# Filler transposes at the start, weights rounded earlier, and VectorE's row maximum moved ahead of the sum of P*V, in a fused attention and two-MLP kernel

## The reference, cut to what matters

```python
scores = scale * q @ k.T                      # 576 x 576 for each of 32 heads
thresh = max(scores, -1) - tau
scores = where(scores >= thresh, scores, -1e9)
attn   = exp(scores - max); attn /= (sum(attn) + 1e-9)
x      = attn @ v                             # then heads side by side: 2304 x 512
h = x @ w_in;  x = (h * sigmoid(1.702 * h)) @ w_out          # first MLP
h = x @ w_in2; out = (h * tanh(softplus(h))) @ w_out2        # second MLP
```

## Time and profile before

| | |
|---|---|
| median of 3 runs | 1164.55 us (1164.22 to 1164.59) |
| the profiled execution's own time | 1164.05 us |
| its span | 1162.3 us |
| granted TensorE clock, mean | 0.995 |
| busy: TensorE matmul / VectorE / ScalarE / GpSimd | 1118.1 / 759.1 / 724.1 / 295.4 us |

### The profile page before, as it was taken

One profiled execution on the slowest core, in us unless ns is written; L12 is line 12 of the kernel. 1 busy time (PEld: TensorE's weight loads), 2 busy tenths in 40 slices (PEclk: granted clock), 3 DMA queues, 4 the chain that ended last, 5 costly groups with the idle time before them and its releaser, 6 DMA issues.

```text
span 1162.3 us, 19359 instructions
## 1 busy us (share of the span) xinstructions
PE 1118.1 (96%) x7472; PEld 1035.4 (89%) x7472; DVE 759.1 (65%) x1359; ACT 724.1 (62%) x995; POOL 295.4 (25%) x502
## 2 busy tenths in 40 slices
PE   8978889999999999999999999999999999999998
PEld 4568889998999999999999999998999989899997
DVE  4678788888888888888888434665433444344343
ACT  3678787767777777777767322467545554554453
POOL 3557674434444433344333000000000000000000
PEclk9989999999999999999999999999999999999999
DMA  2443534232143222233231003520010000000000
GB/s 65 140 131 114 158 86 111 59 94 85 48 111 91 64 82 77 79 105 83 70 103 28 26 19 106 190 76 28 6 49 1 28 28 28 28 28 28 1 28 27
DMA packets 92923, 78.71 MB, mean 68 GB/s; under 512 B 47520, under 2 KB 78752, under 8 KB 92832
## 3 DMA queue, kind: packets, MB, share of 16 engines
q1 hardware_dynamic: 92832, 77.49, 22.9%
HBM read 63.83 MB, written 13.63 MB: 67 GB/s over the span
## 4 chain that ended last, share of the span: by engine, by line
PE 78%; DVE 11%; ACT 7%; issue 3%; POOL 0%; DMA 0%; SPq 0%; ACTq 0%; DVEq 0%
PE ps_s L743 17%; PE ps_r L628 14%; PE ps_r L648 11%; PE ps_r L766 9%; PE ps_t L492 6%; PE ps_t L513 5%; PE ps_t L766 4%; PE ps_s L477 4%; PE ps_t L648 3%; PE ps_r L513 2%; PE ps_s L466 2%; DVE x_pair L585 2%; DVE pt_lo L574 2%; ACT pv_half_sb L544 1%; DVE neg_max L554 1%
## 5 line engine op out<-in xcount | busy, mean ns | idle before, releaser
L628 PE MATMUL ps_r<-x_hi,wi_lo 128*128 128x256 f32 x544 | 158.5, 291 | 2.7 <-DVE x_lo L701 2.7
L810 DVE COPY hidden<-ps_s 128x768 f32<-128x768 f32 x48 | 45.8, 956 | 170.5 <-PE ps_s L743 170.5
L628 PE MATMUL ps_r<-x_lo,wi_hi 128*128 128x256 f32 x544 | 154.2, 284 | 0.0
L628 PE MATMUL ps_r<-x_hi,wi_hi 128*128 128x256 f32 x544 | 154.2, 283 | 0.0
L492 PE MATMUL ps_t<-ident,e_buf 128*128 128x128 f32 x720 | 118.1, 283 | 27.1 <-DVE pt_lo L574 14.5
L839 ACT ACTIVATE m_lo_raw<-m_lo_raw 128x1536 f32<-128x1536 f32 x24 | 35.8, 1491 | 168.8 <-DVE m_lo_raw L817 168.8
L561 DVE SCALAR_TENSOR_TENSOR e_buf<-ps_s,neg_thr,e_buf 128x576 f32<-128x576 f32 x144 | 117.0, 813 | 29.4 <-ACT e_buf L521 22.9
L648 PE MATMUL ps_r<-g_hi,wo_lo 128*128 128x256 f32 x464 | 135.4, 292 | 0.0
L537 ACT CAST pt_hi<-ps_t 128x640 fp32r<-128x640 f32 x128 | 89.0, 695 | 71.8 <-PE ps_t L492 69.6
L743 PE MATMUL ps_s<-x_hi,wi_lo 128*128 128x384 f32 x384 | 129.0, 336 | 2.4 <-DVE x_lo L799 2.4
L492 PEld LDWEIGHTS ps_t<-ident,e_buf 128*128 128x128 f32 x720 | 84.7, 143 | 52.1 <-issue 29.2
(11 more groups left out here) (105 smaller groups left out, 3009.9 us busy)
## 6 DMA issues: line engine op xcount, KB each, us to landing
k_ll_raw<-in_k SPq DMA_DIRECT2D x56, 288.0 KB, 2.9
v_st_raw<-in_v SPq DMA_DIRECT2D x64, 160.0 KB, 2.9
wi_lo_raw<-in_moe_w_in SPq DMA_DIRECT2D x16, 512.0 KB, 3.8
wo_lo_raw<-in_moe_w_out SPq DMA_DIRECT2D x16, 512.0 KB, 4.8
q_raw<-in_q SPq DMA_DIRECT2D x32, 192.0 KB, 2.9
x_scratch<-y_acc SPq DMA_DIRECT2D x9, 512.0 KB, 3.2
x_lo_raw<-x_scratch SPq DMA_DIRECT2D x6, 768.0 KB, 4.7
out_rows<-rows_out SPq DMA_DIRECT2D x18, 256.0 KB, 2.1
```

Of the source, the lines that this page charges most:

```text
L628: mm = pe.matmul(bank[:, part * CH:(part + 1) * CH], wi[w][:, k, f * P:(f + 1) * P], x[:, k, :], start=t == 0, stop=t == 3 * KT - 1)
```

## The change

Six edits:

1. TensorE starts with 12 transposes of the identity onto itself into an unused corner of a PSUM bank, and issues 3 more at the end of each of the turns 0 to 3 (`pe_idle`).
2. The weights' turns move from 9, 12, 14, 17, 19, 21, 23, 24, 26, 28, 30, 31, 33, 34, 36, 37 to 4, 6, 8, 10, 12, 14, 16, 18, 21, 23, 26, 28, 30, 31, 34, 35. The load is issued three turns ahead instead of four. VectorE subtracts the first seven, not four.
3. Chunk 0's first half stands in turn 18, not 19. The plan of turns 20 to 36 shifts by at most one half. From turn 37 it is the same.
4. In turn 18 ScalarE does the P*V copy and the rounding of x before `act_p_hi`.
5. VectorE subtracts the last of the four x blocks in turn 18, not 19.
6. In every turn with a group from 19 on, VectorE takes the maximum of step n before the sum of P*V.

```diff
-READY = [GROUPS[g][4] + (4 if c == 0 else 8) for c, g in enumerate(CHUNK_GROUP)]
+READY = [GROUPS[g][4] + (3 if c == 0 else 8) for c, g in enumerate(CHUNK_GROUP)]
...
-        W_SLOT = dict(zip((9, 12, 14, 17, 19, 21, 23, 24, 26, 28, 30, 31, 33, 34, 36, 37), W_ORDER))
+        W_SLOT = dict(zip((4, 6, 8, 10, 12, 14, 16, 18, 21, 23, 26, 28, 30, 31, 34, 35), W_ORDER))
...
-        W_FIRST = 4
+        W_FIRST = 7
...
+        def pe_idle(pe, count):
+
+            for _ in range(count):
+                pe.transpose(ps_r[:, 1, 384:512], ident[:, :], ident[:, :])
...
             pe.wait_ge(s["ident_ready"], 1)
+            pe_idle(pe, 12)
             pe_scores(pe, 0)
...
+                    if n < 4:
+                        pe_idle(pe, 3)
                     continue
...
-                    if n >= 2:
+                    if 2 <= n < FRONT + 2:
                         act_p_hi(act, n - 2)
...
                         act_x_hi_first(act, X_HI_FIRST[n])
+                    if n == FRONT + 2:
+                        act_p_hi(act, n - 2)
...
+                if 0 <= n < N:
+                    dve_max(dve, n)
                 if n >= FRONT + 3 and n - 3 in GROUP_AT:
                     dve_pv(dve, GROUP_AT[n - 3])
-                if 0 <= n < N:
-                    dve_max(dve, n)
...
-                if n - 1 in X_HI_FIRST:
-                    dve_x_lo_first(dve, X_HI_FIRST[n - 1])
+                for late in (1, 0):
+                    if n - late in X_HI_FIRST and (X_HI_FIRST[n - late] < KT - 1) == (late == 1):
+                        dve_x_lo_first(dve, X_HI_FIRST[n - late])
...
-                if n + 4 in W_SLOT:
-                    w_load(sp, 0, W_SLOT[n + 4])
+                if n + 3 in W_SLOT:
+                    w_load(sp, 0, W_SLOT[n + 3])
```

## The result

The changed kernel is slower: 1171.17 us in the median of 4 runs (1170.8 to 1173.82) against 1164.55 us. The ratio is 1.0064 with a 95% interval of 1.0053 to 1.0076, and the difference is 6.6 us. The profiled execution has a span of 1169.6 us, 7.3 us more than before. I had forecast 1165.6 us, between 1155 and 1173.

What follows compares the result with a forecast made beforehand. From 164 to 640 us TensorE's work plus its waits bound the kernel; the first 164 us hold most idle time. 1164.05 - 4.9 + 4.6 - 2.2 - 5.9 + 9.5 = 1165.15 us, 1165.6 as median; range 1155 to 1173.

Steps and rivals of the forecast that it cites:

- one of its own signs: The prediction is wrong if the first 86 us are not shorter by about 5 us.
- The other sign: From 164 to 640 us TensorE's idle time grows by 7 to 8 us; wrong if that stretch gets no longer.
- Edit 1: Filler transposes at the start lift TensorE's clock, so turn 5 starts at 20.8 us, not 25.66; gain 4.9 us.
- my rival: Transposes do not lift the clock at the start: 4.9 us gain becomes 2.5 us loss, 1173.0 us; chance 0.18.
- mask 0 would end near 9.3 us, mask 3 three loops later: First turns: with the clock up, VectorE's 2.67 us loop sets the pace, and mask 3 ends at 17.3 us.
- Edit 2, the front: Turns 4 to 18: weight roundings behind even turns' P*V delay the next exponential; loss 4.6 us.
- The term for turn 16: Turn 16's weight rounding stands ahead of the norm and copy that turn 18's P*V waits for; loss 1.04 us.
- The middle: Turns 21 to 37: three fewer weights at 0.74 us each; gain 2.2 us.
- Edits 3 to 5: Chunk 0: the 2.67 us wait and the half pace behind it go; gain 5.9 us.
- Edit 6: Maximum before sum delays 32 of 54 sums by 12.6 us, with 3.1 us won back; net loss 9.5 us.

Runs made afterwards that it cites:

- e12: e10 without turn 4's fillers, plus the maximum ahead of the sum only in 27 groups where VectorE had idle time; 1154.1 us, ratio 0.9915 to the kernel before.
- e5: The kernel before with 60 identity transposes ahead of the first scores; one run, 1168.18 us.
- e2: The changed kernel with edit 6 undone, the sum of P*V ahead of the maximum again; 1166.84 us, ratio 1.0032 to the kernel before.
- e3: The changed kernel with edit 2 undone, weights in their old turns and loads four turns ahead; 1166.65 us, ratio 1.0023 to the kernel before.
- e9: e8 with the change's fillers back (12, then 3 in each of turns 0 to 3); 1159.66 us, ratio 0.9963 to the kernel before.
- e10: e8 with fillers: 12 at the start, 12 ending turn 0, 6 ending each of turns 1 to 4; 1154.58 us, ratio 0.992 to the kernel before.
- e6: The kernel before with 40 fp32 matmuls on 64 of 128 rows ahead of the first scores; one run, 1178.21 us.
- e8: e7 with the first eight weights moved to odd turns 5 to 19, no fillers, sum first; 1158.67 us, ratio 0.9954 to the kernel before.
- e7: The kernel before with edits 3 to 5 alone; 1161.66 us, ratio 0.998 to the kernel before.
- e4: The kernel before with edit 6 alone, the maximum ahead of the sum; 1168.96 us, ratio 1.004 to the kernel before.
- e1: The changed kernel without edit 1's filler transposes; 1171.21 us, ratio 1.0058 to the kernel before.

## Why the prediction was right and wrong

The range held the time, in its upper part. The point, 1165.6 us, was no change that a measurement can tell, and 5.6 us too low; I had given slower a chance of 0.36 and faster 0.40. By one of its own signs the prediction failed: the first 86 us were to be about 5 us shorter, and the first sum, which stood at 86.14 us, came 3.4 us later. The other sign held in direction: TensorE's idle time from 164 to 640 us grew, by 4.4 us instead of 7 to 8. The terms one by one:

**Edit 1 is the step that failed.** I had put a gain of 4.9 us; the changed trace has a loss of 1.75 us at turn 5, near the 2.5 us of my rival. In that trace the twelve fillers did not lift the clock (4.18 us for the eight scores), as the rival had it, nor did they in e12's. But the rival's reason, that transposes cannot do it, is wrong. They can: 60 of them in e5, and 12 in the profiled executions of e2, e3, e9 and e10. The changed kernel, e2 and e3 start with the same instructions of TensorE, so the same start goes either way. Work on 64 rows does not lift it: e6 kept it low for 17.4 us, and so the scores are what left it low in the earlier trace rows, most likely. e5 and e6 differ in the operation as well as in the rows, but the P*V, a product on 128 rows, lifts it in every trace where it was low. What I never asked is what holds it. At full pace the scores end sooner, mask 0 does not, and TensorE idles 1.9 us where it had idled 0.73; in e2 and e3 the clock fell in that wait and stayed low until behind the first P*V, 28 us. My step "mask 0 would end near 9.3 us, mask 3 three loops later" took the clock as up, from the first scores on and for good. e10 puts nine more transposes into that gap (and three more into each of the next turns, six into turn 4), and there turn 5 starts at 21.19 us, where the sum had 20.8; e9's one good run had 20.43. That the added fillers are worth 4 us over e8 and 5 over e9 in the median is shown. Whether they do it by ending the idle time, by adding work on 128 rows, or by a second chance to lift the clock (e12) stays open: no run separates these. The Trainium skill's sentence on the PE-mode transpose ("TensorE: Matmul & The Clock Gate"), that it does not count as busy in the same way, is not what e5 shows: the pace of the transposes themselves doubled.

**Edit 2, the front**, had the mechanism right and the size partly by luck: 4.6 us forecast, 4.8 more lag between turn 5 and turn 18. The weights account for 3.6 us of it, the waits named behind turns 4, 6, 8 and 10 (0.84, 0.95, 0.85 and 0.95 more than before). e3 confirms the place and e8 the reason: the same roundings in odd turns cost next to nothing. The term for turn 16, "a full 1.04", was wrong: e3 and e5 have no weight in turn 16, and their P*V of turn 18 waits as long as that of the changed kernel. The rest is chance. In the changed trace the P*V of turn 12 ran at half pace and cost 1.7 us. In the old one that of turn 16 did, and it hid waits behind it:

```profile
62.14 4.06 PE L513 MATMUL ps_r<-pt_hi_raw,v_st_raw 128*64 128x256 f32 x10
...
68.62 2.37 PE L513 MATMUL ps_r<-pt_raw,v_st_raw 128*64 128x256 f32 x10 [0.67 <-ACT pt_raw L537]
```

In e5, whose turns are those of the kernel before behind the 60 fillers, the P*V of turn 16 is fast and the next one waits longer:

```profile
72.30 2.37 PE L513 MATMUL ps_r<-pt_raw,v_st_raw 128*64 128x256 f32 x10 [1.16 <-ACT pt_raw L537]
```

From turn 5 to turn 18 e5 takes 44.70 us and the kernel before 45.27, so the slow P*V of turn 16 cost only 0.6 us, and the two slow ones do not cancel. **The middle** was forecast at 2.2 us. e2 against the kernel before shows 1.6, with edits 3 to 5 in it; e3 against the changed kernel, which differ in the weights alone, shows 0.2.

**Edits 3 to 5** went the way described: no wait of 2.67 us, no fall of the clock there. The size was 5.9 us and turned out 3.1 (lag 6.57 at turn 18, 3.43 at the first sum), 3.2 in e7's trace; e7 gives 2.5 in the median. What I left out is of two kinds. Before the first sum 36 matmuls of the first MLP now stand where 24 stood, which takes one half, 1.4 us, more; and in e7 TensorE waits 0.95 us for the remainder of P in turn 20, where it had not waited. That half is one fewer later on, but e7's lead does not grow behind the first sum. It falls to 1.04 us at 141 us, of which 1.5 us are the fall of the clock at 110 us; why the missing half brings nothing there is not shown.

**Edit 6** had the right sign and mechanism and twice the size: 9.5 forecast, 4.3 in the median by e2 and 4.6 by e4. The mis-sized term is the time that the maximum adds ahead of the sum, 0.66 us and not the 0.77 from start to start; over the 54 sums that makes 9.2 us instead of 12.6. And the order gave back 4.1 us in e4's trace, where I had counted 3.1. Most of the delays came nearly one for one, since TensorE's fifth tile waits for the sum.

So two errors of 5 to 7 us of opposite sign, edit 1 too good and edit 6 too bad, with chunk 0 a further 2.8 us too good, made a point that looked closer than its parts: up to the first sum I had 6.2 us won and the trace lost 3.4, behind it I had 7.3 lost and the trace lost 3.9. That the time lies in the range owes something to this.

## What to carry to other kernels

A filler that lifts TensorE's clock is worth only what holds it afterwards: work out where TensorE will wait once it is faster, and put fillers there too. Before a difference of 1 to 2 us between two traces is put down to the change, look for stretches at half pace in either: one P*V at half pace is 1.7 us. Before moving work on an in-order engine, look at what the instruction ahead of it waits for: the same 1.04 us costs 0.85 us behind a late wait and nothing a turn away (e8, turns 5 to 13). Putting work into an idle gap ahead of an instruction that another engine waits for costs, at each place, its length less the gap there, so count the gaps one by one and move it only where it fits.

## What the runs showed of the hardware that was not expected

fp32 matmuls on 64 of 128 rows, 17.4 us of them without a gap, left TensorE at the 1.2 GHz level, while identity transposes on 128 rows brought it to 2.4 GHz near 5 us from the start (e5, 60 of them). Twelve of them, 2.82 us of work, did it in four of six profiled executions (e2, e3, e9, e10) and not in two (the changed kernel, e12). The granted clock's column reads 1.00 in these first microseconds even while the matmuls keep the lower level's pace (before, changed kernel, e5, e6); there only the distance between starts tells. A wait of 1.5 to 1.9 us for mask 0 after the clock had come up was followed by the lower level in three of the profiled executions (e2 1.86 us, e3 1.67, e5 1.68) and not in a fourth (e9, 1.54 us). Later in the kernel, too, the clock fell for a few microseconds at places that differ from trace to trace: 0.58 and 0.56 in the windows from 110 to 114 us in e7, none there in e8. Executions of one kernel lie up to 7 us apart, with fillers (e9, 1153.74 to 1160.8 us) and without (e1, 1168.53 to 1175.41); how much of that is the clock only the profiled ones could show.
